# The negated bias of a masked softmax: one tensor and a pointer scalar in place of two tensor inputs

## The chip, the cores and the metric

The kernel runs on one core of one Trainium2 chip. The metric is the device time of one launch, in microseconds (us). Engines are called PE (TensorE, matmuls), DVE (VectorE), ACT (ScalarE), POOL (GpSimd) and SP (SyncE, here a DMA queue). SBUF is the memory that all engines read, PSUM the one that PE writes.

## What is computed

A block of bucketed attention, then a mixture of experts with two of eight experts per token, then a dense layer with a rational activation. Only the first part bears on the change:

```python
scores = scale * np.matmul(q, k.transpose(0, 1, 3, 2))   # 2 x 8 heads, 768 x 768, head size 64
scores = np.where(mask, scores, -1000000000.0)           # mask: same bucket of 6 random signs
scores = scores - np.max(scores, axis=-1, keepdims=True)
attn = np.exp(scores)
attn = attn / (np.sum(attn, axis=-1, keepdims=True) + 1e-09)
return np.matmul(attn, v).astype(np.float32)
```

## The kernel before, in words

Each engine has a stream of instructions of its own, written out by hand, and semaphores order them. The whole is one pipeline of three stages: attention (here called the attention stage), routing with the experts' matmuls, and the dense layer.

**Attention.** The 16 heads are worked through as 8 pairs (n = 0 to 7; head A and head B of a pair, `hh` 0 and 1). A pair has T = 6 steps (t = 0 to 5), each for 128 query rows of both heads. Pairs 1 to 4 are a hardware loop of two bodies, pairs 0, 5, 6 and 7 are written out (`pairs`, L357). Where this text speaks of a step of a pair, it is the time from one maximum of head A (L1263) to the next.

In a step the engines do this, one block of rows after the other:

- PE (`PE_STEP`, L53): turns an earlier output (L1013), makes the scores of A and of B in PSUM (L979, L980, 768 columns each), transposes the exponentials of the step before (L988), and multiplies those of two steps before by the values (L1001). In some steps it also makes the bucket bits of the next pair (L963 to L967), one of them at a time, in the one PSUM bank `ps_m`.
- DVE (`DVE_STEP`, L55): divides an earlier output by its sum (`normalise`: den L1275, rinv L1277, lg_head L1283, x_sb L1287), then `softmax` for head A, then one half of the bits of the next pair (L1252 or L1255), `softmax` for head B, bits again, and `turn_tile` (L1241).
- `softmax` (L1258) is three instructions: the row maximum `mx` out of PSUM (L1263, 128 x 768 to 128 x 1), the scale `sc` (L1265, 128 x 1: SSCALE or 0, by whether the maximum says that the row has a match), and the negated bias `nb` = -mx x sc (L1268, 128 x 1). Each waits for the one before through a semaphore. `mx`, `sc` and `nb` are tiles of four fp32 columns in SBUF.
- ACT (`ACT_STEP`, L54): copies the transposed exponentials (L744), makes the exponential of A and of B from the scores with `nb` as bias and `sc` as scale (`exp`, L751), copies the output (L756), and rounds a tile of the next pair (`round_tile`, L784).
- POOL (`tiles`, L582): for each of the four tiles (q and k of both heads) of the next pair it makes the low parts. For q these are L593 (tile_t times a constant, 64 x 768), L596 (minus the high part) and L580 (a copy), for k L600. Then it splits a chunk of the first expert's weights (L574, 128 x 1024, called `first_split`). All of them have two tensor inputs in SBUF.

The next pair's tiles pass through one buffer, `tile_t`. DVE's `turn_tile` fills it in steps 0, 1, 2 and 3 (last in the step, `TURN_AT`); ACT rounds it at the start of the following step (`ROUND_AT`); POOL takes the low part; and before DVE fills it again, it waits for `tile_split`, which L596 (q) or L600 (k) signals:

```python
if not (isinstance(n, int) and n * NTILES + r == 0):
    dve.wait_ge(tile_split, n * NTILES + r)
dve.transpose(tile_t[:].rearrange("p (t a j) -> p t a j", t=T, a=Q), ...
```

So turn_tile of step 1 waits for the q tile that ACT rounds at the start of step 1.

**After attention.** The last rows are routed (L1307 to L1343), scattered to memory by POOL (L642), gathered again by ACT's queue (L825), and the experts' matmuls begin (L1106).

Of the kernel before, what the change touches and what calls it, by code (L numbers as in the profile page):

```python
# [14 lines left out]
ALU = mybir.AluOpType  # L15
# [42 lines left out]
def fused_kernel(nc, q, k, v, proj, w_gate, w_noise, noise, w1, w2, w_in, w_out, a, b, out):  # L58
# [33 lines left out]
    def small(name, shape, dt):  # L92
        n = 4 if dt != BF else 2
        for s in shape[1:]:
            n *= s
        t = at(name, c[0], shape, dt)
        c[0] += (n + 31) // 32 * 32
        return t
# [3 lines left out]
    mx = small("mx", [P, 4], F)  # L102
    sc = small("sc", [P, 4], F)
    nb = small("nb", [P, 4], F)
# [91 lines left out]
    def sem(name):  # L196
        if name not in sems:
            sems[name] = nc.alloc_semaphore(name)
        return sems[name]
# [23 lines left out]
    soft_ready = [sem("soft_readyA"), sem("soft_readyB")]  # L223
# [186 lines left out]
    with nc.Block() as block:  # L410
# [794 lines left out]
        def _(dve):  # L1205
# [52 lines left out]
            def softmax(n, t, hh):  # L1258

                i = 2 * (t % 2) + hh  # L1260
                e = n * T + t + 1
                dve.wait_ge(scored[hh], e)
                dve.tensor_reduce(mx[:, i:i + 1], ps_s[hh][:, 0:S], AX.X, ALU.max).then_inc(row_max_done[hh], 1)  # L1263
                dve.wait_ge(row_max_done[hh], e)
                dve.tensor_scalar(sc[:, i:i + 1], mx[:, i:i + 1], -0.25, SSCALE, ALU.is_gt,  # L1265
                                  ALU.mult).then_inc(scale_done[hh], 1)
                dve.wait_ge(scale_done[hh], e)
                dve.scalar_tensor_tensor(out=nb[:, i:i + 1], in0=mx[:, i:i + 1], scalar=-1.0, in1=sc[:, i:i + 1],  # L1268
                                         op0=ALU.mult, op1=ALU.mult).then_inc(soft_ready[hh], 1)

            def normalise(n, t, last):
                e = n * T + t + 1
# [109 lines left out]
            def steps(n, half, par, first, last):  # L1382
                for t in range(T):
                    for what in DVE_STEP:
                        if what == "A max":
                            softmax(n, t, 0)
                        elif what == "B max":
                            softmax(n, t, 1)
                        elif what == "output" and not (first and t < 3):
                            m, _, u = back(n, par, t - 3)  # L1390
                            normalise(m, u, False)
                        elif isinstance(what, int):
                            point(n, par, t, what, last)
                if last:
                    turned_out(n, T - 2, 1)
                    normalise(n, T - 3, last)
                    turned_out(n, T - 1, 0)
                    logits(*GROUPS[2])
                    add_noise(2)
                    best(2)  # L1400
                    which(2)
                    choose(2)
                    normalise(n, T - 2, last)
                    normalise(n, T - 1, last)
                    logits(*GROUPS[3])
                    place(2)
                    add_noise(3)
                    best(3)
                    which(3)
                    choose(3)  # L1410
                    place(3)
# [7 lines left out]
            def over(z, n, where):  # L1419
# [9 lines left out]
                                          op0=ALU.mult, op1=ALU.add),  # L1429
# [19 lines left out]
                                          op0=ALU.mult, op1=ALU.subtract),  # L1449
                 dve.scalar_tensor_tensor(out=full[:, 2, :], in0=full[:, 0, :], scalar=-float(P), in1=region[:],  # L1450
                                          op0=ALU.add, op1=ALU.add),
# [166 lines left out]
```

## Time and profile before

| | us |
|---|---|
| median of 3 runs | 1004.0 (1003.65 to 1005.6) |
| the profiled execution | 1007.57 |
| its span | 1006.0 |
| busy: PE | 916.6 (91%) |
| busy: PE weight load | 787.0 (78%) |
| busy: DVE | 604.2 (60%) |
| busy: ACT | 498.1 (50%) |
| busy: POOL | 470.9 (47%) |
| mean granted clock of PE | 0.973 |

The profile is of one execution; times in it are from the start of its span. A row of a timeline gives the start, the duration, engine, line, operation and `out<-in` with the tiles' names without buffer numbers, then, in brackets, how long the engine had been idle and who released it. Releasers are inferred from semaphore events. An operation that is held up inside itself shows no idle time but a longer duration.

### The profile page before, as it was taken

What the parts mean: (1) busy time and instruction counts of PE and PEld (TensorE: products, weight loads), DVE (VectorE), ACT (ScalarE), POOL (GpSimd) and SP (SyncE); (2) the same over time, 40 slices, a digit from 0 to 9 for tenths busy, and PEclk for the clock granted to TensorE, in tenths of its full rate; (3) what the DMA queues carried; (4) which work ended last, traced back from release to release, by engine and by line L of the source; (5) the groups of instructions that cost most, each with busy time, mean ns of one, the idle gap of its engine ahead of it and who ended that gap; (6) DMA issues with size and microseconds to landing.
All of it is one profiled execution on the core that took longest, in us unless ns stands there. A gap on an engine that the chain in (4) does not pass through costs nothing.

```text
span 1006.0 us, 17834 instructions
## 1 busy us (share of the span) xinstructions
PE 916.6 (91%) x5505; PEld 787.0 (78%) x5506; DVE 604.2 (60%) x1229; ACT 498.1 (50%) x886; POOL 470.9 (47%) x373
## 2 busy tenths in 40 slices
PE   6799899989792799999999999998489999999998
PEld 5677777777682588888888888887479999999997
DVE  7799899989967222322222222221388877887775
ACT  3577677677571122222222222221367777777775
POOL 4624544352444455655472635610576555453222
PEclk9899999999996899999999999999689999999999
DMA  9952643453133868777886758823621110110000
GB/s 201 257 179 80 153 102 91 109 131 96 64 116 137 261 196 264 250 233 240 279 259 220 245 176 281 283 98 107 199 84 44 41 53 22 53 32 9 33 1 32
DMA packets 88149, 143.63 MB, mean 143 GB/s; under 512 B 15522, under 2 KB 47778, under 8 KB 87586
## 3 DMA queue, kind: packets, MB, share of 16 engines
q1 hardware_dynamic: 46450, 72.19, 24.0%
q0 software_dynamic: 19328, 54.53, 17.0%
q10 hardware_dynamic: 22320, 16.26, 5.4%
q8 instruction: 28, 0.46, 0.2%
q14 instruction: 23, 0.19, 0.1%
HBM read 123.30 MB, written 19.66 MB: 142 GB/s over the span
## 4 chain that ended last, share of the span: by engine, by line
PE 67%; DVE 11%; issue 10%; POOL 7%; ACT 2%; DMA 2%; SPq 2%; ACTq 0%; another core or an unknown queue 0%; DVEq 0%; POOLq 0%
PE ps_s L1106 17%; PE ps_o L1131 17%; PE ps_s L1174 13%; PE ps_t L1160 6%; DVE mx L1263 4%; PE ps_s L1160 3%; PE ps_m L1160 3%; PE ps_s L1117 3%; DVE nb L1268 1%; POOL qs L596 1%; PE ps_t L988 1%; DVE tile_t L1241 1%; PE ps_o L1001 1%; POOL tile_t L593 1%; POOL w_r L574 1%
## 5 line engine op out<-in xcount | busy, mean ns | idle before, releaser
L553 POOL TENSOR_TENSOR w_r<-raw,w_r 128x1024 f32 (+1 forms) x72 | 171.9, 2404 | 107.5 <-DMA raw<-in_moe_w 48.1
L1106 PE MATMUL ps_s<-w_r,xT 128*128 x744 | 178.7, 396 | 17.0 <-DVE xT L1477 17.0
L1131 PE MATMUL ps_o<-w_r,hT 128*128 x744 | 174.0, 389 | 2.6 <-DVE hT L1481 2.6
L1106 PEld LDWEIGHTS ps_s<-w_r,xT 128*128 128x128 f32 x744 | 138.5, 189 | 45.1 <-issue 17.2
L1131 PEld LDWEIGHTS ps_o<-w_r,hT 128*128 128x128 f32 x744 | 139.6, 188 | 31.7 <-issue 2.8
L1174 PE MATMUL ps_s<-w_r,g_r 128*128 128x512 f32 x576 | 145.9, 398 | 4.8 <-DVE g_r L1563 4.8
L1487 DVE COPY y_sb<-ps_o 128x512 f32<-128x512 f32 x31 | 21.4, 692 | 209.9 <-PE ps_o L1131 209.9
L1174 PEld LDWEIGHTS ps_s<-w_r,g_r 128*128 128x128 f32 x576 | 107.7, 190 | 25.5 <-issue 4.6
L692 POOL TENSOR_TENSOR m<-q,g_r 128x384 f32<-128x384 f32 x64 | 65.2, 1019 | 114.9 <-DVE g_r L1551 114.7
L751 ACT ACTIVATE prob<-ps_s,nb,sc 128x768 f32<-128x768 f32 x96 | 95.1, 991 | 47.2 <-DVE nb L1268 47.0
L836 ACT ACTIVATE hT<-ps_s 128x1024 fp32r<-128x1024 f32 x31 | 31.8, 1026 | 160.3 <-DVE y_sb L1487 111.1
L1263 DVE TENSOR_REDUCE mx<-ps_s 128x1 f32<-128x768 f32 x96 | 91.4, 952 | 2.6 <-PE ps_s L980 1.2
L744 ACT ACTIVATE probT<-ps_t 128x768 f32<-128x768 f32 x93 | 75.2, 808 | 31.8 <-PE ps_t L988 30.5
L988 PE MATMUL ps_t<-ident,prob 128*128 128x128 f32 x570 | 80.0, 277 | 1.3 <-ACT probT L744 1.0
L979 PE MATMUL ps_s<-km,qm 128*128 128x512 f32 x192 | 72.3, 380 | 4.0 <-ACT prob L751 2.2
L1001 PE MATMUL ps_o<-probT,v_in 128*64 128x128 f32 x1128 | 72.3, 277 | 0.8 <-DVE x_sb L1287 0.6
L1160 PE MATMUL ps_t<-x2T,w_r 128*128 (+1 forms) x384 | 72.3, 337 | 0.0
L593 POOL TENSOR_TENSOR tile_t<-tile_t,qscale 64x768 f32<-64x768 f32 x14 | 20.5, 1465 | 107.1 <-ACT qs L784 107.1
L1160 PEld LDWEIGHTS ps_t<-x2T,w_r 128*128 128x128 f32 x384 | 68.2, 188 | 2.6
L1529 DVE SCALAR_TENSOR_TENSOR v<-s,ab,t 128x384 f32<-128x384 f32 x64 | 45.8, 715 | 38.1 <-ACT t L891 38.0
L988 PEld LDWEIGHTS ps_t<-ident,prob 128*128 128x128 f32 x570 | 63.9, 141 | 5.9 <-issue 4.8
L1001 PEld LDWEIGHTS ps_o<-probT,v_in 128*64 128x64 f32 x1128 | 61.1, 137 | 8.8 <-issue 8.7
(245 smaller groups left out, 1540.7 us busy)
## 6 DMA issues: line engine op xcount, KB each, us to landing
w_r<-in_moe_w POOLq DMA_DIRECT2D x32, 1024.0 KB, 8.5
raw<-in_moe_w SPq DMA_DIRECT2D x56, 512.0 KB, 3.9
q_in<-in_q SPq DMA_DIRECT2D x56, 176.0 KB, 3.5
k_in<-in_k SPq DMA_DIRECT2D x56, 176.0 KB, 4.4
xg<-x_slots ACTq DMA_DIRECT2D x124, 64.0 KB, 3.3
y_slots<-y_sb ACTq DMA_DIRECT2D x31, 256.0 KB, 4.5
raw<-in_moe_w SPq DMA_DIRECT2D x16, 256.0 KB, 2.9
raw<-in_moe_w_in SPq DMA_DIRECT2D x8, 512.0 KB, 5.2
```

The costliest lines, as they stand in the source:

```text
L553: pool.tensor_tensor(of_chunk(buf, 1, n), raw[:, par, :], of_chunk(buf, 0, n).bitcast(F), ALU.subtract).then_inc(split_done, 1)
L692: pool.tensor_tensor(m2[:], q2[:, f % 2, :], g_r[:, f % 4, 0, :].bitcast(F), ALU.mult).then_inc(m_ready, 1)
L744: act.activation(probT[:, hh, t % 2, :], src[:, 0:S], ACT.Copy).then_inc(pt_ready[hh], 1)
L751: act.activation(prob[:, hh, t % 2, :], ps_s[hh][:, 0:S], ACT.Exp, bias=nb[:, i:i + 1], scale=sc[:, i:i + 1], accum_out=rs[:, hh, t:t + 1] ...
L979: pe.matmul(o, qm[:, par, hh, rows], km[:, par, hh, c0:c1], start=True, stop=False)
L988: mm = pe.transpose(to[:, u * P:(u + 1) * P], prob[:, hh, t % 2, u * P:(u + 1) * P], ident[:])
L1001: mm = pe.matmul(to[64 * hh:64 * hh + 64, 0:P], v_in[:, par, hh, u * D:(u + 1) * D], probT[:, hh, t % 2, u * P:(u + 1) * P], start=(u == 0 ...
L1106: mm = pe.matmul(ps_s[0][:, o * 512:o * 512 + 512], xT[:, par, part, c * P:c * P + P], w_r[:, buf, wpart, col:col + 512], start=(c == 0 an ...
L1131: mm = pe.matmul(ps_o[:, :], hT[:, part, c * P:c * P + P], w_r[:, buf, wpart, col:col + DM], start=(c == 0 and part == 0 and wpart == 0), ...
L1160: mm = pe.matmul(ps_a[f % 4], w_r[:, 0, wpart, c * FF2 + f * P:c * FF2 + f * P + P], x2T[:, par, part, c, :], start=(c == 0 and wpart == 0 ...
L1174: mm = pe.matmul(ps_b[j], g_r[:, f % 4, part, j * P:j * P + P], w_r[:, 1, wpart, f * DM:f * DM + DM], start=(f == 0 and part == 0 and wpar ...
L1263: dve.tensor_reduce(mx[:, i:i + 1], ps_s[hh][:, 0:S], AX.X, ALU.max).then_inc(row_max_done[hh], 1)
```

## The change

The bias is written by a `tensor_scalar` with two operations (by the pointer scalar `sc`, then by -1.0) in place of a `scalar_tensor_tensor` whose second tensor is `sc`. The waits ahead of it, the signal behind it and the result's place are the same.

```diff
                 dve.wait_ge(scale_done[hh], e)
-                dve.scalar_tensor_tensor(out=nb[:, i:i + 1], in0=mx[:, i:i + 1], scalar=-1.0, in1=sc[:, i:i + 1],
-                                         op0=ALU.mult, op1=ALU.mult).then_inc(soft_ready[hh], 1)
+                dve.tensor_scalar(nb[:, i:i + 1], mx[:, i:i + 1], sc[:, i:i + 1], -1.0, ALU.mult,
+                                  ALU.mult).then_inc(soft_ready[hh], 1)
```

## Rows read from the trace of the kernel before

**Rows 1.** Attention: stretch, length, busy PE, PEld, DVE, ACT, POOL, clock, DMA, GB/s.
```profile
17.00:310.00 293.00, 257.07 (x2329) 219.05 (x2328) 252.64 (x611) 201.48 (x368) 130.89 (x87) 0.99 0.46 129
```

**Rows 2.** The same view, step 5 of pair 3.
```profile
158.46:163.47 5.01, 5.01 (x49) 4.46 (x48) 4.52 (x14) 3.93 (x8) 0.00 (x0) 1.00 0.30 93
```

**Rows 3.** List of groups, DVE: count, busy us, mean ns, idle us before.
```profile
L1268 DVE SCALAR_TENSOR_TENSOR nb<-mx,sc 128x1 f32<-128x1 f32 x96 | 45.1, 470 | 3.3
...
L1275 DVE TENSOR_SCALAR den<-rs 128x2 f32<-128x2 f32 x48 | 9.8, 204 | 0.4
```

**Rows 4.** Durations of one line's instructions: least/median/most, first and last start.
```profile
L1268 DVE SCALAR_TENSOR_TENSOR nb<-mx,sc x96: 158/160/1918, 19.3 to 301.7; 128x1 f32<-128x1 f32 x96
...
L1265 DVE TENSOR_SCALAR sc<-mx x96: 153/154/155, 19.1 to 301.5; 128x1 f32<-128x1 f32 x96
```

**Rows 5.** Timeline of DVE and POOL, step 1 of pair 2.
```profile
98.16 1.47 POOL L593 TENSOR_TENSOR tile_t<-tile_t,qscale 64x768 f32<-64x768 f32 x1 [12.29 <-ACT qs L784]
98.19 1.46 DVE L1268 SCALAR_TENSOR_TENSOR nb<-mx,sc 128x1 f32<-128x1 f32 x1
...
99.70 1.81 POOL L596 TENSOR_TENSOR qs<-tile_t,qs 64x768 fp32r<-64x768 f32 x1
...
100.55 0.15 DVE L1265 TENSOR_SCALAR sc<-mx 128x1 f32<-128x1 f32 x1
100.73 0.80 DVE L1268 SCALAR_TENSOR_TENSOR nb<-mx,sc 128x1 f32<-128x1 f32 x1
101.55 0.98 DVE L1241 STREAM_TRANSPOSE tile_t<-k_in 128x768 f32<-128x768 f32 x1
...
102.45 0.70 DVE L1275 TENSOR_SCALAR den<-rs 128x2 f32<-128x2 f32 x1
```

**Rows 6.** Durations of two lines, and a stretch of the dense layer's timeline.
```profile
L1255 DVE TENSOR_SCALAR km<-ps_m,thr x29: 606/615/616, 13.2 to 271.7; 32x384 fp32r<-32x384 f32 x29
...
L1252 DVE TENSOR_SCALAR qm<-ps_m x28: 555/555/556, 34.8 to 264.6; 32x384 fp32r<-32x384 f32 x28
...
783.60 2.40 POOL L553 TENSOR_TENSOR w_r<-raw,w_r 128x1024 fp32r<-128x1024 f32 x1 [0.49 <-DVE v L1529]
...
784.43 0.61 DVE L1541 SCALAR_TENSOR_TENSOR ps_m<-p,ab,ps_m 128x384 f32<-128x384 f32 x1
```

**Rows 7.** L1268 alone: stretch, length, busy; step 1 of pairs 2 and 5.
```profile
97.00:103.83 6.83, 2.26 (x2) 1.00 0.41 119
...
203.54:210.31 6.77, 0.44 (x2) 1.00 0.41 112
```

**Rows 8.** Timeline of DVE, step 1 of pair 5.
```profile
208.25 0.98 DVE L1241 STREAM_TRANSPOSE tile_t<-k_in 128x768 f32<-128x768 f32 x1 [2.00 <-POOL qs L596]
```

**Rows 9.** Busy us of L1268 alone, step 2: pair 0, and pairs 0 to 6.
```profile
31.88:39.05 7.17, 1.87 (x2) 0.77 1.20 341
...
sum 45.86, DVE 8.37; mean DVE 1.20
```

**Rows 10.** Timeline of DVE and POOL, steps 3 and 4 of pair 3.
```profile
149.86 1.46 POOL L580 TENSOR_TENSOR qm<-qs,nought 64x768 fp32r<-64x768 f32 x1
...
151.44 0.13 DVE L1275 TENSOR_SCALAR den<-rs 128x2 f32<-128x2 f32 x1
...
154.60 2.38 POOL L574 TENSOR_TENSOR w_r<-raw,w_r 128x1024 f32 x1 [0.30 <-POOL km L600]
...
157.61 0.17 DVE L1275 TENSOR_SCALAR den<-rs 128x2 f32<-128x2 f32 x1
```

**Rows 11.** Busy us of L1268: steps 3 and 4, pairs 0-6; step 5, pair 6.
```profile
sum 45.75, DVE 5.26; mean DVE 0.75
...
sum 44.13, DVE 11.23; mean DVE 1.60
...
266.54:273.04 6.50, 2.08 (x2) 1.00 0.32 115
```

**Rows 12.** Chain of work that ended last, first expert matmuls.
```profile
332.35 7.26 PE ps_s L1106 x24
```

## The prediction

> **What bounds the kernel now.** I first split the span by stage. In the attention stage (17 to 310 us) DVE is busy 252.6 us of 293 and PE 257.1, so neither has much room [rows 1]; the changed line runs only here. The chain of waits through pairs 1 to 4 goes from one DVE instruction to the next in steps 2, 3 and 4 of a pair, and through PE in steps 5 and 0. So a microsecond of DVE in steps 2 to 4 should be a microsecond of the kernel, while in steps 5 and 0 PE has work all the time: 5.01 us of the 5.01 us of step 5 [rows 2].
>
> Next the line itself. The list of groups gives 45.1 us for its 96 instructions, a mean of 470 ns [rows 3]. By their durations they last 158 ns at least, 160 in the median and 1918 at most, while the scale just before, of the same 128x1 shape, takes 153 to 155 in all 96 cases [rows 4]. A one-column operation that takes 160 ns in the median and 470 in the mean is waiting inside itself. The timeline of step 1 of pair 2 shows for what [rows 5]: nb starts at 98.19, 0.03 us after the L593 of POOL, and ends at 99.65 where that ends (99.63). The second nb starts at 100.73 and ends at 101.53, with POOL's L596 (101.51). It is so for all 96: each one over 300 ns overlaps a POOL tensor operation and ends within 0.03 us of its end. The scale at 100.55, in the middle of L596, still takes 0.15. What tells the two apart is the second SBUF tensor that nb reads. The waits are worth 45.1 - 96 x 0.16 = 29.7 us of DVE.
>
> **The change, part by part.** It removes 96 STT instructions and adds 96 tensor_scalar instructions at the same place, behind the same two waits, with the same signal. No DMA, semaphore or queue order moves.
>
> Price of the new instruction: the trace has no 128x1 operation with a pointer scalar from SBUF. Lower bound: the scale's 154 ns. Upper bound: what a pointer adds where the rest is alike, 615 ns (pointer threshold) against 555 (immediate) on 32x384, so 60 more: 214 ns [rows 6]. I take 210, the dearer end, since that pair of rows is the nearest. That is 50 ns more than an undisturbed nb has now, 96 x 0.05 = 4.8 us if all of it counted.
>
> Does it still wait for POOL? At 784.43 an STT with one SBUF tensor, one PSUM tensor and an SBUF pointer runs wholly inside a POOL operation (783.60 to 786.00) and takes 0.61 [rows 6], its usual time. So neither one SBUF tensor nor the pointer waits. I take no wait.
>
> There is one DVE operation of this kind that does wait: den (128x2, immediate) starts at 102.45 inside L580, which follows L596, and ends with it, 0.70 us [rows 5] in place of 0.13 [rows 10]. The single-column scale doesn't [rows 4, 5]. The Trainium skill (VectorE: DVE Perf Modes, "Mode 2×_2P") says a tensor_scalar with source and destination in SBUF uses both read ports if the outermost non-unit dimension is even, or is equal for source and destination; the page SBUF — State Buffer ("Who interferes with whom") says such an instruction and GpSimd shut each other out. By that rule the new nb could wait as the old one does, and the sum would be the cost of the pointers alone; the trace agrees with it for two columns and not for one.
>
> Where does DVE time come free? I sum the line's busy time over the same step of pairs 0 to 6 (an undisturbed pair of nb is 0.32, the new one 0.42).
>
> Step 1: nb takes 2.26 us in a step of 6.83 (four such pairs, one with 2.16) [rows 7]. But behind both nb stands turn_tile (L1241), which overwrites tile_t and so waits for POOL's L596. It started at 101.55, right at the end of nb, and L596 ended at 101.51 [rows 5]. With nb short, the first ends at 98.19 + 0.21 = 98.40, the second starts 1.08 later as it does now (100.73 after 99.65) and ends at 99.69, and DVE stands from 99.7 to the same 101.53. Pair 5 shows the case already: there the two nb take 0.44 and the step still takes 6.77 [rows 7], because turn_tile idles 2.00 behind L596 [rows 8]. So the 9.6 us that step 1 seems to hold are worth 0: the stall passes from L1268 to L1241. The den that follows is still caught by L580.
>
> Step 2: here nb of head A overlaps L600, and nothing on DVE asks for L600 until turn_tile at the end of the step, when it is long done; PE's next bits matmul and both exponentials wait for DVE and move with it. 8.37 us in all; in pair 0 (1.87) the granted clock is 0.77, between the levels of 1.2 and 2.4 GHz, and PE is busy throughout, so I count it at nothing [rows 9]. The other six: 8.37 - 1.87 - 12 x 0.21 = 4.0 us.
>
> Step 3: 5.26 us in all [rows 11]. But the den behind it begins at 151.44, only 0.12 after the end of L580 (149.86 + 1.46) [rows 10], and is itself an operation that waits for POOL. DVE can come forward by some 0.12 before den catches the wait that nb gave up. Two pairs (1 and 3) get 0.12, pair 5 about 0.15, the even ones nothing beyond that (their nb lost 0.1); pair 0 then waits for the DMA of k_in, and in pair 6 the two-tensor sum at L1319 is still held by L580. 0.4 us.
>
> Step 4: 11.23 us in all [rows 11], gross (11.23 - 14 x 0.21) / 7 = 1.2 per pair. But L574 runs from 154.60 to 156.98 and den, at 157.61 now, would come at about 156.3, inside it [rows 10]. It would then end at about 157.01 in place of 157.78: 0.77 for each of seven pairs, 5.4 us.
>
> Step 5: only pair 6 has a wait, 2.08 us of nb in 6.50 [rows 11]; PE's 5.01 us per step [rows 2] leaves 1.5. Steps 5 and 0 of the other pairs pay 0.05 more for each nb under a busy PE: nothing, at most 26 x 0.05 = 1.3 us.
>
> From the end of attention to the first expert matmul (332.35) everything is one chain of waits (routing, scatter, gather), and from there PE runs without a gap [rows 12], so what attention gains is kept.
>
> Sum: 0 + 4.0 + 0.4 + 5.4 + 1.5 = 11.3 us. The profiled execution took 1007.57 (span 1006.0), 3.6 above the median of 1004.0; I take the difference off both: 996.3 profiled, median about 993.
>
> **The rivals.**
> A. All the waits come back as time: 29.7 - 4.8 = 25 us, about 979. For it: the chain runs through DVE and the stage gets shorter in many places at once, and earlier ACT work lets POOL's own tile operations start earlier. Against it: the stall of 2.00 in pair 5, and den's 0.70.
> B. Little comes back: nb's waits in steps 2 and 4 are replaced as in step 1, by PE. In step 2 PE's bits matmul waits for DVE now, which speaks against it, but PE already fills 257 of 293 us. Half of step 2 and a fifth of step 4 would be left, less the pointers: 0 to 4 us, 1000 to 1004.
> C. Slower: the new instruction is held by POOL as den is at 102.45, or its pointer is fetched as the second tensor is now. Then all waits stay and each nb costs 0.05 more: 4.8 us, less the third of it that lies in steps 5 and 0: 3.2 us, about 1007. It decides if more than a few new nb exceed 0.3 us. Against it: 0.61 at 784.43 and 0.15 at 100.55. This is also the case in which the change doesn't do what its form promises.
>
> **How the numbers follow.** Forecast 0.74, A 0.08, B 0.12, C 0.06. A measurement of this kernel can tell about 0.2%, 2 us, from no change. The forecast and A are faster, 0.82; B splits into 0.05 faster and 0.07 same; C into 0.01 same and 0.05 slower: 0.87, 0.08, 0.05. The likeliest time is 993. For the range: if den does not wait in step 4 and step 3 gives its full 1.8, 4 to 5 us more come back; with 154 ns for the new instruction the 28 of steps 2 and 3, some 1.5; and part of step 1 might; that leads from 993 to 983. If PE keeps half of steps 2 and 4 and steps 5 and 0 pay, 6 to 8 us are lost: 1001. Outside lie most of A, the upper part of B and C, some 0.2.
>
> **What the profile would show.** Right: 96 TENSOR_SCALAR for nb, all between 150 and 220 ns; idle time of about 1.8 us before L1241 from POOL's L596 in step 1 of each pair; step 1 still about 6.8 us long, step 2 shorter by 0.7 and step 4 by 0.7; den's busy time up from 9.8 us [rows 3] by 3 to 4, its longest cases inside L574; the stage from 332 us on unchanged. Wrong: nb above 0.3 us (C); step 1 down by a microsecond or more (A); new idle time of DVE before a bits operation, released by PE, of the size of the saving (B); a den that stays at 0.13 in step 4 would make my sum 3 to 4 us too small.

## The result, and the profile after

The changed kernel takes 990.27 us in the median of 4 runs (988.26 to 992.4), the one before 1003.83 beside it: a ratio of 0.9865, interval 0.9834 to 0.9896, or 13.6 us less. On another chip, with 5 runs and more runs of before, the ratio was 0.9851 (0.9834 to 0.9869). The profiled execution took 992.4 us, with a span of 990.8 against 1006.0. 993 had been forecast.

First the changed line and the two lines to which it was thought to pass its wait, from the list of groups of DVE (count, busy us, mean ns, idle us before) of the kernel after:

```profile
L1268 DVE TENSOR_SCALAR nb<-mx,sc 128x1 f32<-128x1 f32 x96 | 20.6, 214 | 3.4
L1241 DVE STREAM_TRANSPOSE tile_t<-k_in 128x768 f32<-128x768 f32 x14 | 13.7, 979 | 17.8 <-POOL qs L596 16.4 <-DMA k_in<-in_k 1.3
L1275 DVE TENSOR_SCALAR den<-rs 128x2 f32<-128x2 f32 x48 | 12.9, 270 | 0.4
```

nb falls from 45.1 us to 20.6, but den rises from 9.8 to 12.9 [rows 3], and turn_tile (L1241) stands 16.4 us behind POOL's L596 (5.8 of them in pair 0, where it had stood 6.6 before). The durations of the line (least, median, most) leave no doubt that the wait itself is gone:

```profile
L1268 DVE TENSOR_SCALAR nb<-mx,sc x96: 212/214/216, 18.9 to 286.3; 128x1 f32<-128x1 f32 x96
```

Against [rows 4] the most has gone from 1918 ns to 216 and the least has risen from 158 to 212. 40 of the 96 lie wholly inside one of POOL's tensor operations and still take their 0.21 us. The timeline of DVE and POOL in step 1 of pair 2, the same place as [rows 5], shows both halves of that in one picture:

```profile
94.66 1.47 POOL L593 TENSOR_TENSOR tile_t<-tile_t,qscale 64x768 f32<-64x768 f32 x1 [11.50 <-ACT qs L784]
94.67 0.21 DVE L1268 TENSOR_SCALAR nb<-mx,sc 128x1 f32<-128x1 f32 x1
...
95.97 0.21 DVE L1268 TENSOR_SCALAR nb<-mx,sc 128x1 f32<-128x1 f32 x1
96.20 1.83 POOL L596 TENSOR_TENSOR qs<-tile_t,qs 64x768 fp32r<-64x768 f32 x1
98.06 0.98 DVE L1241 STREAM_TRANSPOSE tile_t<-k_in 128x768 f32<-128x768 f32 x1 [1.87 <-POOL qs L596]
98.17 1.46 POOL L580 TENSOR_TENSOR qm<-qs,nought 64x768 fp32r<-64x768 f32 x1
98.96 0.70 DVE L1275 TENSOR_SCALAR den<-rs 128x2 f32<-128x2 f32 x1
```

nb starts 0.01 us into L593 and is done in 0.21. The second one is done at 96.18, and then DVE stands 1.87 us until L596 ends at 98.03. POOL is where it was: L596 starts 2.71 us after the step does, 2.70 before.

The same with the busy time of the engines, step 0 to step 5 of pair 3 (stretch, length, busy us of PE, PE weight load, DVE, ACT and POOL, granted clock, DMA share, GB/s):

```profile
123.29:127.94 4.65, 4.65 (x47) 4.09 (x46) 4.17 (x13) 3.49 (x8) 0.00 (x0) 1.00 0.00 0
127.94:134.80 6.86, 6.60 (x58) 5.54 (x56) 4.66 (x11) 5.73 (x11) 5.11 (x4) 1.00 0.38 109
134.80:140.52 5.72, 5.23 (x47) 4.57 (x48) 5.28 (x14) 4.18 (x8) 1.46 (x1) 1.00 0.87 190
140.52:146.51 5.99, 5.86 (x54) 5.03 (x53) 5.55 (x15) 4.79 (x9) 4.75 (x3) 1.00 0.47 120
146.51:151.80 5.29, 5.03 (x47) 4.18 (x45) 4.85 (x13) 3.87 (x8) 4.19 (x2) 1.00 0.55 136
151.80:156.79 4.99, 4.80 (x47) 4.16 (x47) 4.55 (x13) 3.44 (x7) 0.00 (x0) 1.00 0.31 105
```

In step 1 DVE is busy 4.66 of 6.86 us: the step has the old length with a DVE that is idle in it. The last step compares with [rows 2]: 4.99 against 5.01. These are steps 1, 2 and 4 of the same pair before the change:

```profile
132.79:139.61 6.82, 6.33 (x55) 5.16 (x54) 6.49 (x11) 5.40 (x10) 4.73 (x3) 1.00 0.38 108
139.61:146.05 6.44, 5.61 (x53) 4.78 (x52) 6.00 (x14) 4.61 (x9) 1.81 (x1) 1.00 0.78 171
152.25:158.46 6.21, 4.95 (x45) 3.99 (x44) 5.77 (x14) 3.66 (x8) 4.19 (x2) 1.00 0.50 126
```

Where the time came from, with the lengths of the steps (from one maximum of head A, L1263, to the next) summed over pairs 1 to 6, whose steps repeat within a few hundredths of a us in the second profile of the changed kernel:

| step | before | after | difference | forecast for six pairs |
|---|---|---|---|---|
| 0 | 28.18 | 28.30 | +0.12 | 0 |
| 1 | 40.72 | 40.68 | -0.04 | 0 |
| 2 | 38.69 | 34.75 | -3.94 | -4.0 |
| 3 | 38.97 | 37.02 | -1.95 | -0.4 |
| 4 | 38.18 | 32.99 | -5.19 | -4.6 |
| 5 | 31.36 | 29.73 | -1.63 | -1.5 |
| all | 216.10 | 203.47 | -12.63 | -10.5 |

The rest of the difference of the two spans (15.2 us) lies in the start, in pair 0, in one step of pair 7 and between the last pair and the experts, places that differ by 1 to 3 us from one execution to the next: pair 0 took 38.83 us before, 37.66 in this profile and 38.89 in the second profile of the same changed kernel. One part of pair 0 does repeat: its step 4 took 5.95 us before and takes 5.20 in both profiles of the changed kernel. With it 13.4 us are accounted for.

### The profile page after: what moved, and what is told of

Same layout as the page of the kernel before. It is cut to its first block, busy times and chain, and to the rows that moved or that the text cites. A ratio compares the mean times of both kernels' runs of the same rounds, so it can differ in the third digit from the quotient of the medians.

```text
span 990.8 us, 17834 instructions
## 1 busy us (share of the span) xinstructions
PE 917.7 (93%) x5505; PEld 789.8 (80%) x5506; DVE 583.7 (59%) x1229; ACT 497.5 (50%) x886; POOL 471.8 (48%) x373
## 4 chain that ended last, share of the span: by engine, by line
PE 68%; DVE 10%; issue 9%; POOL 7%; ACT 2%; DMA 2%; SPq 2%; ACTq 0%; DVEq 0%; POOLq 0%
PE ps_s L1106 17%; PE ps_o L1131 17%; PE ps_s L1174 13%; PE ps_t L1160 6%; DVE mx L1263 3%; PE ps_s L1160 3%; PE ps_m L1160 3%; PE ps_s L1117 3%; POOL qs L596 1%; PE ps_t L988 1%; POOL tile_t L593 1%; POOL w_r L574 1%; DVE tile_t L1241 1%; PE ps_o L1001 1%; DMA raw<-in_moe_w_out 1%
## 5 line engine op out<-in xcount | busy, mean ns | idle before, releaser
L1263 DVE TENSOR_REDUCE mx<-ps_s 128x1 f32<-128x768 f32 x96 | 91.3, 951 | 3.0 <-PE ps_s L980 1.6
L1001 PE MATMUL ps_o<-probT,v_in 128*64 128x128 f32 x1128 | 72.0, 276 | 3.4 <-DVE x_sb L1287 3.2
L1529 DVE SCALAR_TENSOR_TENSOR v<-s,ab,t 128x384 f32<-128x384 f32 x64 | 48.1, 752 | 37.9 <-ACT t L891 37.6
L1001 PEld LDWEIGHTS ps_o<-probT,v_in 128*64 128x64 f32 x1128 | 61.0, 137 | 11.6 <-issue 11.5
L593 POOL TENSOR_TENSOR tile_t<-tile_t,qscale 64x768 f32<-64x768 f32 x14 | 20.5, 1466 | 101.3 <-ACT qs L784 101.2
```

What stands on the lines that cost most here:

```text
L1001: mm = pe.matmul(to[64 * hh:64 * hh + 64, 0:P], v_in[:, par, hh, u * D:(u + 1) * D], probT[:, hh, t % 2, u * P:(u + 1) * P], start=(u == 0 ...
```

## The experiments

All ratios are against the kernel before on the same chip, with 95% intervals. The second reading of the changed kernel went with the first set.

> The changed kernel beside the others on one chip. Every theory: 0.986 to 0.990 of the kernel before, nb at 212 to 216 ns in all 96 cases. It gives the ratio that the other runs of this set are held against.

Measured: 992.99 us, 0.9851 (0.9834 to 0.9869), just below the 0.986 to 0.990 expected; nb 213 to 216 ns. The kernel before took 1008.69 us on that chip, so the difference of the medians is 15.7 us.

### Is it the second SBUF tensor that waits, or the instruction?

```diff
-dve.tensor_reduce(mx[:, i:i + 1], ps_s[hh][:, 0:S], AX.X, ALU.max)
+dve.tensor_reduce(ps_s[hh][:, 1020:1021], ps_s[hh][:, 0:S], AX.X, ALU.max)
...
-dve.scalar_tensor_tensor(out=nb[:, i:i + 1], in0=mx[:, i:i + 1], scalar=-1.0, in1=sc[:, i:i + 1],
+dve.scalar_tensor_tensor(out=nb[:, i:i + 1], in0=ps_s[hh][:, 1020:1021], scalar=-1.0, in1=sc[:, i:i + 1],
```

(The scale reads the maximum from the same PSUM column.)

> The kernel before, with its scalar_tensor_tensor for nb kept, but mx in a spare column of the scores' PSUM tile, so that only one of the two tensor inputs is in SBUF. Theory (the second SBUF tensor waits for POOL): no nb over 0.3 us though the instruction is the old one, and about the time of the changed kernel, 988 to 994 for a kernel before of 1004. Rival (the form scalar_tensor_tensor waits, or the saving came from something else in the new form): nb keeps its 29 us of waits, mean about 470 ns, and the time stays at 1002 to 1006.

Measured: 992.66 us, 0.984 (0.9824 to 0.9856). The durations of the line in this kernel:

```profile
L1268 DVE SCALAR_TENSOR_TENSOR nb<-ps_s,sc x96: 157/157/160, 18.9 to 286.4; 128x1 f32<-128x1 f32 x96
```

and from its list of groups the one that waits longer instead, as den does in the changed kernel:

```profile
L1275 DVE TENSOR_SCALAR den<-rs 128x2 f32<-128x2 f32 x48 | 13.4, 280 | 0.4
```

The old instruction, with one of its tensors moved to PSUM, never waits, and the whole gain is there. The rival falls. So for this instruction it was the second tensor in SBUF that waited, and not its form. The run also gives a price for the pointer: 214 against 157 ns for the same product, 57 ns. The two differ in form and in where the maximum lies, so this is a difference of two ways and not a pointer alone; the scale, a tensor_scalar of the same shape in SBUF with immediates, takes 153 to 156 in the changed kernel, which makes it some 60.

### Does a tensor_scalar escape the wait in every shape?

```diff
-dve.tensor_scalar(nb[:, i:i + 1], mx[:, i:i + 1], sc[:, i:i + 1], -1.0, ALU.mult, ALU.mult)
+dve.tensor_scalar(nb[:, 2 * i:2 * i + 2], mx[:, 2 * i:2 * i + 2], sc[:, i:i + 1], -1.0, ALU.mult, ALU.mult)
```

(`mx` and `nb` have eight columns; each second one is zero and not used.)

> The changed kernel with mx and nb two columns wide (the second column is zero and not used), else the same tensor_scalar with the same pointer. Theory (a tensor_scalar of two SBUF columns is held by POOL as den is): nb waits again, its busy time goes from 20.6 us to 45 to 52, and the time is 1002 to 1008. Rival (the pointer form never waits, den's wait has another cause): nb stays near 0.21 us and the time at 988 to 994.

Measured: 1008.53 us, 1.001 (0.9996 to 1.0024). The whole gain is gone with one more column. The list of groups (this kernel's lines lie one further on) and step 1 of its timeline:

```profile
L1269 DVE TENSOR_SCALAR nb<-mx,sc 128x2 f32<-128x2 f32 x96 | 52.2, 543 | 3.4
```

```profile
97.90 1.46 POOL L593 TENSOR_TENSOR tile_t<-tile_t,qscale 64x768 f32<-64x768 f32 x1 [12.31 <-ACT qs L784]
97.92 1.47 DVE L1269 TENSOR_SCALAR nb<-mx,sc 128x2 f32<-128x2 f32 x1
```

nb ends at 99.39 where L593 ends (99.36), as in [rows 5]. So rival C of the prediction, "held by POOL as den is", was a near thing: it is false for one column and true for two. It also limits what the run before said: here only one tensor input lies in SBUF, and the instruction waits all the same. The Trainium skill (VectorE: DVE Perf Modes, "Mode 2×_2P") gives as the condition of the mode that uses both ports that the outermost non-unit dimension is even, or odd and equal for source and destination. The trace agrees with its first half: den and this nb have two columns and wait. An nb of one column has no non-unit dimension, so the prediction stretched the rule when it let it cover that case; the 96 durations of 212 to 216 ns say that one column isn't held. An odd number above one was not run.

### What became of the waits that nb gave up: den

```diff
-dve.tensor_scalar(den[:, :, t], rs[:, :, t], 1e-9, None, ALU.add).then_inc(den_done, 1)
-dve.wait_ge(den_done, e)
-dve.reciprocal(rinv[:, t, :], den[:, :, t]).then_inc(rinv_done, 1)
+dve.reciprocal(rinv[:, t, :], rs[:, :, t]).then_inc(rinv_done, 1)
```

> The changed kernel without den (L1275, the addition of 1e-9 to a sum that is at least 1, which changes no bit of it): rinv is made from the sum itself. Theory (den catches part of the waits that nb gave up, behind L580 in step 1 and 3 and behind L574 in step 4): per pair 0.73 off step 1, 0.16 off step 2, 0.16 to 0.3 off step 3, 0.4 to 0.6 off step 4, nothing in steps 5 and 0, so about 1.6 for each of six pairs, 9 to 10 us less than the changed kernel. Rival (these waits are covered by other work, only the instruction's own 0.16 counts in steps 1 to 4): 3 to 4 us less. Second rival (DVE is not what sets the steps any more): within 1 us.

Measured: 982.92 us, 0.9739 (0.9723 to 0.9755), 10.1 us less than the changed kernel on that chip. By steps of pairs 1 to 6: step 1 from 40.68 to 36.37, step 2 to 33.61, step 3 to 35.44, step 4 from 32.99 to 29.48; step 5 goes up by 0.9 to 30.63. In pair 3 that step lasts 5.21 us and PE is busy for all of them (4.80 of 4.99 in the changed kernel), so more of PE's work falls there. Both rivals (3 to 4 us, and 1 us) fall. This is what the wait of den looked like in the changed kernel, steps 3 and 4 of pair 3, the place of [rows 10]:

```profile
144.34 1.46 POOL L580 TENSOR_TENSOR qm<-qs,nought 64x768 fp32r<-64x768 f32 x1
145.56 0.26 DVE L1275 TENSOR_SCALAR den<-rs 128x2 f32<-128x2 f32 x1
...
148.72 2.38 POOL L574 TENSOR_TENSOR w_r<-raw,w_r 128x1024 f32 x1 [0.30 <-POOL km L600]
...
150.52 0.60 DVE L1275 TENSOR_SCALAR den<-rs 128x2 f32<-128x2 f32 x1
```

den had begun 0.12 us after L580; now it begins 0.24 before its end (145.80) and takes 0.26. Behind L574 (end 151.10) it takes 0.60, to 151.12. In its place the reciprocal, of two SBUF columns too, stands at 97.22 inside L580 (96.43 to 97.89) and isn't held, in the kernel without den:

```profile
96.43 1.46 POOL L580 TENSOR_TENSOR qm<-qs,nought 64x768 fp32r<-64x768 f32 x1
97.22 0.12 DVE L1275 RECIPROCAL rinv<-rs 128x2 f32<-128x2 f32 x1
```

The same edit on the kernel before tells whether the two waits are one:

> The kernel before (two SBUF tensors for nb) without den. Theory (nb and den share one wait: whichever comes first into the POOL operation takes it): here nb still takes it, so what den gives up before an nb that ends with POOL's operation is swallowed by that nb. Left are 0.16 per step where no POOL wait follows, in all 2 to 5 us less than the kernel before. Rival (the two are independent): the 10 us that the same edit gave in the changed kernel.

Measured: 1002.6 us, 0.9988 (0.9977 to 0.9998): 1.3 us, even less than the 2 to 5 of the theory, and far from the rival's 10. Step 1 does lose its den (40.72 to 36.34 over six pairs), and step 2 gives 2.75 of those 4.4 back (38.69 to 41.44), step 5 another 1.1 (PE is busy all through it here too, 5.22 of 5.22 us in pair 3). The timeline of step 2 of pair 2 shows where:

```profile
103.98 1.81 POOL L600 TENSOR_TENSOR km<-tile_t,kh 64x768 fp32r<-64x768 f32 x1 [1.04 <-ACT kh L784]
104.04 1.77 DVE L1268 SCALAR_TENSOR_TENSOR nb<-mx,sc 128x1 f32<-128x1 f32 x1
```

nb arrives earlier at the same L600 and waits 1.77 in place of 0.99. So two edits that are worth 1.3 us and 15.7 us alone are worth 25.8 together (medians beside the kernel before on the same chip; ratios 0.9988, 0.9851 and 0.9739). With one of them alone, the time that it frees brings the other instruction earlier to an operation of POOL: without nb's wait den is caught by the same L580 or L574, without den the next nb is caught by L600.

### What a microsecond of DVE is worth

```diff
 dve.tensor_scalar(nb[:, i:i + 1], mx[:, i:i + 1], sc[:, i:i + 1], -1.0, ALU.mult, ALU.mult).then_inc(soft_ready[hh], 1)
+dve.tensor_scalar(nb_spare[:, i:i + 1], mx[:, i:i + 1], sc[:, i:i + 1], -1.0, ALU.mult, ALU.mult)
```

> The changed kernel with each nb instruction issued twice, the second into a spare tile that nothing reads; it follows without a wait, so DVE gets some 0.1 to 0.2 us more per nb, 10 to 20 us over 96. Theory (step 1 has a stall of 1.9 us behind L596, steps 3 and 4 have den waiting for POOL, steps 5 and 0 have PE full; only step 2 pays in full): 1 to 4 us slower than the changed kernel, step 1 stays at 6.85. Rival (each us of DVE is a us of the kernel): 9 to 20 us slower.

Measured: 993.17 us, 0.9885 (0.987 to 0.99), beside 0.9865 and 0.9851 for the changed kernel on its two chips: 2.0 to 3.4 us more. From its timeline, the second instruction starts 0.13 after the first and ends 0.12 after it:

```profile
97.47 0.21 DVE L1269 TENSOR_SCALAR nb<-mx,sc 128x1 f32<-128x1 f32 x1
97.60 0.20 DVE L1271 TENSOR_SCALAR nb_spare<-mx,sc 128x1 f32<-128x1 f32 x1
99.43 0.98 DVE L1242 STREAM_TRANSPOSE tile_t<-k_in 128x768 f32<-128x768 f32 x1 [1.63 <-POOL qs L597]
```

96 times 0.12 us is 11.5 us of DVE, and a sixth to a third of it shows. In step 1 the stall shrinks from 1.87 to 1.63, and the step keeps its length. The rival, 9 to 20 us, falls. The steps of pairs 1 to 6 add up to 2.4 us more. Of these, step 2 has 1.2, nearly the full 1.4 of its 12 instructions, as the theory had it; but step 5 pays 1.1 and steps 3 and 4 together 0.6 where the theory said nothing, and steps 0 and 1 give 0.5 back.

### What sets step 1

```diff
-TURN_AT = {(0, 2): 0, (1, 2): 1, (2, 2): 2, (3, 2): 3}
-ROUND_AT = {(1, 0): 0, (2, 0): 1, (3, 0): 2, (4, 0): 3}
+TURN_AT = {(0, 1): 0, (1, 2): 1, (2, 2): 2, (3, 2): 3}
+ROUND_AT = {(0, 2): 0, (2, 0): 1, (3, 0): 2, (4, 0): 3}
```

> The changed kernel with the first tile of a pair turned between the two maxima of step 0 and rounded by ACT in step 0 instead of at the start of step 1, so that POOL's L593 and L596 begin about 1.5 to 2 us earlier. Theory (the end of L596 sets the length of step 1): the idle time of L1241 behind L596 goes from 17 us to under 5, step 1 from 6.85 to 5.0 to 5.6, step 0 grows by 0.2 to 1.0 because the rounding now stands ahead of B's exponential; net 3 to 10 us faster than the changed kernel. Rival (step 1 is long because its other work, PE or ACT, is long): the stall goes but the step stays within 0.3 of 6.85 and the time within 2 us.

Measured: 988.79 us, 0.9844 (0.983 to 0.9857), at best 2 us less than the changed kernel: in time a miss. The idle time of L1241 behind L596 is 7.8 us, not under 5, but nearly all of it (7.6) is in pair 0; in pairs 1 to 6 it is gone. And step 1 fell from 6.85 to 5.40 in every pair of the loop, and step 0 did not grow at all (28.26 against 28.30). What took it back is step 2, up from 5.72 to 7.07 in pair 3 and from 6.08 to 7.70 in pair 2. The timeline of pair 2, with SP's queue:

```profile
99.17 0.98 DVE L1241 STREAM_TRANSPOSE tile_t<-k_in 128x768 f32<-128x768 f32 x1
...
99.86 0.88 SPq L422 DMA_DIRECT2D v_in<-in_v  x2
100.92 1.79 SPq L436 DMA_DIRECT2D q_in<-in_q  x4
...
107.31 0.98 DVE L1241 STREAM_TRANSPOSE tile_t<-q_in 128x768 f32<-128x768 f32 x1 [1.36 <-DMA q_in<-in_q]
```

The first tile was turned long before 99.17, yet the load of q_in for the third tile is issued only at 100.92: on SP it stands behind the wait for the previous pair's last values (L1001), after which v is loaded. The next run moves it ahead of that wait:

```diff
-if not first:
-    sp.wait_ge(pv_done, n * T)
-    load_v(n + 1, 1 - par)
 for r in range(NTILES):
...
     load_tile(n + 1 + r // 2, (r + 2) % NTILES)
+    if r == 0 and not first:
+        sp.wait_ge(pv_done, n * T)
+        load_v(n + 1, 1 - par)
```

> As the run with the first tile turned early, and SP's queue now issues the load of that tile's successor before it waits for the pair's last values and loads v. There step 1 had gone from 6.85 to 5.40, but turn_tile of step 2 stood 1.1 to 1.4 us for the DMA of q_in, since its load sat on SP behind that wait. Theory: the DMA wait of step 2 goes, step 2 falls from about 7.1 to 5.7 to 6.1, step 1 stays at 5.4, and the time is 6 to 9 us below the changed kernel (0.976 to 0.981 of the kernel before). Rival (the time only moves on to another wait, POOL's L600 or PE): within 3 us of the changed kernel.

Measured: 983.24 us, 0.9796 (0.9776 to 0.9816), 5 to 7 us less than the changed kernel by its two ratios, and inside the ratio that was forecast. The wait for the DMA is gone, step 1 is 5.36 to 5.39 in pairs 1 to 5, and step 2 is 6.02 in pair 3, 0.30 longer than in the changed kernel: there DVE now waits 0.31 for PE's bits (L964). So the end of L596 did set the length of step 1, with some 1.5 us per pair, and about 0.3 of it moves on to PE.

### Together, and the price of the pointer

> The maximum in PSUM with the old scalar_tensor_tensor (157 ns, no wait), and no den. Theory (the pointer's 57 ns were hidden in part because den caught the gain): against the changed kernel without den the two nb of steps 2, 3 and 4 now count, 36 x 0.057 = 2 us less, 0.971 to 0.973 of the kernel before. Rival (the 57 ns are never on the path): equal within 1 us to the changed kernel without den, 0.974.

Measured: 977.86 us, 0.9745 (0.9729 to 0.9762): by the ratio no better than 0.9739 with the pointer, which is what the rival said, though the steps of pairs 1 to 6 are 1.6 us shorter (193.44 and 191.88). Since the chips of the two sets differ, both kernels were run again on one:

> The changed kernel without den, again, on one chip with the next, to price the pointer. Both theories: 0.973 to 0.976 of the kernel before.

> The maximum in PSUM (nb at 157 ns) and no den, again. If the pointer's 57 ns count in steps 2 to 4: 1.5 to 2 us below the run before it. If they never count: equal within 0.5 us.

Measured: 981.12 us, 0.9773 (0.9754 to 0.9792) with the pointer, 979.08 us, 0.9742 (0.9724 to 0.976) without it. The intervals just overlap; the steps of pairs 1 to 6 add up to 193.39 and 192.05 us. So the 57 ns, 5.5 us over 96, cost 1.3 us by these steps and 2 by the medians, and the whole times alone do not set it apart from zero. With den in place the same comparison of steps (the changed kernel, and the one with the maximum in PSUM) had given 203.47 and 202.01, 1.5 us. In sum den did not hide the pointer's price, it only moved it: steps 2, 3 and 4 hold 1.0 of it with den and 1.3 without, step 5 holds 0.4 and 0.1, and steps 0 and 1 hide it in both. These are differences of a few tenths from one profile each.

> All together: maximum in PSUM with the old scalar_tensor_tensor, no den, first tile turned early, its successor's load ahead of v. If the parts add: 10 us of den and 7 us of the early tile, some less because the 0.7 us of den in step 1 lay behind the same POOL chain: 0.960 to 0.967 of the kernel before. If they overlap fully: 0.973, as without den alone.

Measured: 978.23 us, 0.9737 (0.972 to 0.9755): the lowest ratio that was run, but level with 0.9742 and 0.9739 without the early tile. The gains did not add: that would have been 0.960 to 0.967. The busy time of the engines from 60 to 220 us, in the kernel before, the changed one, and the maximum in PSUM without den (this last one from its second run):

```profile
60.00:220.00 160.00, 145.75 (x1319) 123.80 (x1318) 144.41 (x324) 116.49 (x211) 71.73 (x42) 1.00 0.44 112
```

```profile
60.00:220.00 160.00, 152.23 (x1376) 130.53 (x1375) 137.06 (x340) 120.96 (x217) 77.54 (x45) 1.00 0.46 118
```

```profile
60.00:220.00 160.00, 159.05 (x1478) 138.27 (x1478) 134.31 (x335) 128.14 (x233) 77.98 (x46) 1.00 0.46 120
```

PE goes from 145.75 to 152.23 to 159.05 of 160 us, DVE from 144.41 down to 134.31. After den is gone PE has almost no room left, and with the early tile DVE waits 0.96 us in step 1 for PE's L1013 where it had waited 1.9 for POOL in the changed kernel:

```profile
95.81 0.47 PE L1013 MATMUL ps_o<-turn_w,oT 128*128 x2
96.50 0.19 DVE L1281 TENSOR_TENSOR lg_head<-ps_o,rinv 128x32 f32 x1 [0.96 <-PE ps_o L1013]
```

## Why the prediction was right

**What the change removes.** 29.7 us of waits inside nb, by [rows 3, 4]: all of them went, and the second tensor in SBUF was the cause, as the run with the maximum in PSUM shows. That the new form would escape came true as well, but "neither one SBUF tensor nor the pointer waits" was too wide: it rested on an instruction that reads PSUM too [rows 6], and with two columns one SBUF tensor is enough to wait. What carried it was the scale, of one column as nb is [rows 5].

**Price of the new instruction.** 214 ns, the upper bound, worked out from two lines of 32x384 [rows 6]; I used 210. The upper bound was the value. That bound came from a pair of rows of another shape; that the price would carry over was luck in part.

**Step 1, 9.6 us of waits worth nothing.** Borne out: -0.04 us over six pairs, with 1.87 us of idle time in place of the 1.8 forecast. This was the costliest step to get wrong, and one row, the 2.00 us of pair 5 [rows 8], told it. The early tile shows that L596 is the cause.

**Step 2.** 4.0 forecast, 3.94 measured.

**Step 3.** This is the term that was mis-sized: 0.4 forecast, 1.95 measured. 1.36 of it is pair 6. I wrote that "the two-tensor sum at L1319 is still held by L580". In the profile after, DVE gets there sooner and L1319 begins before L580 does; it is another two-tensor operation, L1318, that is caught by the tail of L596:

```profile
242.87 1.82 POOL L596 TENSOR_TENSOR qs<-tile_t,qs 64x768 fp32r<-64x768 f32 x1
244.84 1.49 POOL L580 TENSOR_TENSOR qm<-qs,nought 64x768 fp32r<-64x768 f32 x1
```

```profile
244.19 0.56 DVE L1318 TENSOR_TENSOR noisy<-sp,noise_sb 128x48 f32<-128x48 f32 x1
244.79 0.21 DVE L1319 TENSOR_TENSOR noisy<-noisy,lg 128x48 f32<-128x48 f32 x1
```

L1319 had taken 1.36 us and takes 0.21, while L1318 goes from 0.21 to 0.56, and the first nb of the step gives up its 0.61. Before, L1319 had begun 0.16 us after L580; now it begins 0.05 us ahead of it and keeps its time, and L580 takes 1.49 in place of 1.46. An offset that small turns round when DVE comes forward, so it should not have been carried over. In pairs 1, 3 and 5 the 0.12 to 0.15 per pair became 0.2: POOL's L580 ends where it did (5.27 us into step 3 of pair 3 before, 5.28 after), but I counted only the gap ahead of den. den's own 0.13 us now falls inside the wait too, so that it ends 5.30 us into the step in place of 5.52.

**Step 4.** 0.77 per pair forecast from where den would land in L574; measured 0.93, 0.78, 0.92, 0.76, 1.10 and 0.70 in pairs 1 to 6, and 0.75 in pair 0. In pair 3 the surplus is POOL's: L574 starts 2.21 us into the step, 2.35 before. den's busy time was to rise by 3 to 4 us and rose by 3.1. The kernel without den shows that these waits were real time.

**Step 5 and the rest.** 1.5 forecast and 1.65 measured in pair 6; nothing lost in steps 0 and 5 elsewhere (+0.12 and +0.02).

The rivals: A (all waits come back) misses the stall behind L596 and den. It would have needed 25 us. The changed kernel without den is 25.8 us below, but that takes a second instruction away, so it isn't A come true. B (PE takes the place) came only once DVE had shed more. C's condition falls for one column and holds for two; there the ratio is 1.001 (0.9996 to 1.0024), level with before, where C had 3.2 us more.

The sum was too low: 11.3 us were forecast and 13.6 (medians beside each other) or 15.7 (second chip) measured. The steps that repeat hold 13.4: the 12.6 of pairs 1 to 6 and 0.75 of pair 0. What is over the forecast there is step 3 (1.6) and the surplus of step 4 (0.6). What lies beyond 13.4 stays open: pair 0, the start and the passage to the experts scatter too much between profiles to be told apart.

## What to carry to other kernels

When small DVE operations have a mean far above their median, lay their ends beside the ends of POOL's operations: if they coincide, count the tensors that they read from SBUF, and take one away (a pointer scalar, or a PSUM column). The pointer form helps only where it isn't caught itself: here it ran free with one column and waited with two. The PSUM column was tried with one. Before adding up such waits, ask of each what DVE does next: one that another instruction waits for anyway, or that the next operation of the same kind would catch, is worth nothing until that one is gone too. When several instructions can be caught by POOL one after the other, try their removals together; one at a time each is worth less than its share.

## What was not expected of the hardware

- A tensor_scalar from SBUF to SBUF with one column (nb, 96 times 212 to 216 ns; the scale, 153 to 156) is not held by POOL, with two columns (nb 228 to 1907, den 125 to 698) it is, and a reciprocal with two columns (122 to 169) isn't.
- A pointer scalar costs some 57 to 60 ns on a 128x1 operation, as much as the 60 ns on 32x384 [rows 6]. Over these two shapes it is a fixed price and not one per element.
- A second, independent DVE instruction straight behind the first adds 0.12 us, though each lasts 0.20.
